# Four experts, four orders: how the second and first products of a mixture of experts are woven on TensorE

## The chip, the core and the metric

The kernel runs on one core of a Trainium2 chip. The metric is the device time of one execution in microseconds. Everything below the section on the profile is taken from one execution recorded by the hardware profiler.

## What is computed

Three stages follow one another: a gated linear attention, a bilinear layer, and a mixture of four experts. Cut to what matters:

```python
def reference(q, k, v, alpha, w1, w2, w3, w_out, domain_probs, e_w1, e_w2):
    for t in range(768):                       # batch 4, heads 8, head_dim 48
        state = alpha_t * state + outer(k_t, v_t)
        y_t = q_t @ state
    x = y as (3072 tokens, 384)
    x = ((x @ w1) * (x @ w2)) @ w3 @ w_out     # inner width 1024
    p = domain_probs / (domain_probs.sum(-1) + 1e-9)
    out = 0
    for e in range(4):                         # the part that the change touches
        h = maximum(x @ e_w1[e], 0)            # 384 -> 1024
        out += p[:, e] * (h @ e_w2[e])         # 1024 -> 384
```

## The kernel before, in words

**Stages.** The attention and the bilinear layer take the first 414 us. The rest, some 800 us, are the experts, and only they are changed.

**Tiling of the experts.** The 3072 tokens are six tiles of 512. For each expert (a Python loop over 4) the tiles are taken two at a time in three rounds; the first two rounds are the body of a loop on the engine (`pe.Fori`), the third is written out. A round has 16 steps: two tiles, and for each the eight blocks of 128 of the inner width. All values are fp32, and each product is made of three: every operand is split into a high and a low part, and high x high, one low x high and the other high x low are added up in the same bank of PSUM.

**The first product (line 1175, `up2_product`), "U" below.** For one tile and one block of 128 inner columns: 3 blocks of the model width by 3 terms, 9 matmuls of 512 columns. They gather in bank 0 or 1 by the step's parity. The ninth releases ScalarE, which writes `h_hi` as the relu (line 601), and that releases VectorE, which writes `h_lo`, the rest (line 821).

**The second product (line 1294, `down2_product`), "D" below.** For the same tile and block: four groups of 128 tokens by 3 terms, 12 matmuls of 384 columns. Group `sub` gathers in bank 5, 2, 3 or 4 (`SUM_BANKS`; bank 5 is one of `score_banks` in the profile's names) over the eight steps of a tile. After the last, VectorE multiplies by the gate and adds to `total` (line 1000), and counts up `added`; the first D of the next tile in that bank waits for it (line 1291).

**The order (line 1299, `step2`).** Step s makes the D of block s and, in between, the U of step s + 2, so that ScalarE and VectorE have a whole step for h. TensorE waits at the head of a step for `h_lo` of the step, and at a tile's first block for the loaded activations (`up2_waits`). Within the step the Python loop writes D number i and, where i % 4 is 1, 2 or 3, a U behind it. As there are 12 D and 9 U, the step is three times the same seven: D D U D U D U. Read as a ring (the seventh is followed by the first), such a pattern of four D and three U can take five different forms. The last two steps of all have no U.

**Other engines.** ScalarE and POOL also split the weights of the next expert in pieces; the queue on SP loads activations and weights, each load behind a count of finished U or D, and stores `total` during the last expert. Their code is not changed.

Of the kernel before, what the change touches and what calls it, by code (L numbers as in the profile page):

```python
# [31 lines left out]
BATCH, HEADS, SEQ, D = 4, 8, 768, 48  # L32
# [11 lines left out]
KT, FT = DM // P, FF // P  # L44
# [11 lines left out]
SUBS = TILE2 // P  # L56
# [9 lines left out]
FOLD_BANKS = [0, 1, 2, 3, 4, 0, 1, 2]  # L66
SUM_BANKS = [5, 2, 3, 4]
TERMS = 3
assert KT * TERMS == SUBS * TERMS - TERMS
WARM = 6  # L70
CONSTANTS = 7
FLAG_STEP = STEPS1 - 4
# [16 lines left out]
def gated_attention_experts(nc, akq, v, akq_long, v_columns, w3T, w_out, wsets, probs, out):  # L89
# [4 lines left out]
    with ExitStack() as ctx:  # L94
# [924 lines left out]
        def _(pe):  # L1019
# [143 lines left out]
            def up2_waits(e, m, s):  # L1163
                u, f = divmod(s, FT)
                if f == 0:
                    pe.wait_ge(x1_loaded[u], 32 * (e * ROUNDS + m + 1))
                    if u == 0 and isinstance(m, int) and m == 0:
                        pe.wait_ge(piece_lo, PIECES * (e + 2))

            def up2_product(e, s, i):  # L1170

                u, f = divmod(s, FT)
                k, term = divmod(i, TERMS)
                cols = slice(k * FF + f * P, k * FF + (f + 1) * P)
                mm = pe.matmul(bank[s % 2][:, :], (we_hi if term < 2 else we_lo)[e % 2][:, cols], (x1_lo if term == 1 else x1_hi)[u][:, k, :],  # L1175
                               start=(i == 0), stop=(i == KT * TERMS - 1))
                if i == KT * TERMS - 1:
                    mm.then_inc(up_done, 1)
# [36 lines left out]
            for k in range(FT):  # L1215
# [5 lines left out]
                for f in range(FOLD_FIRST):  # L1221
# [5 lines left out]
                    else:  # L1227
                        i = k - SPLIT_FROM
# [55 lines left out]
            def down2_product(e, m, s, i):  # L1284

                u, f = divmod(s, FT)
                sub, term = divmod(i, TERMS)
                if term == 0 and e == 0 and s == 0 and sub >= 1:
                    pe.wait_ge(x1_lo_ready, X1_LOW_AHEAD + KT * (TILES1 * BATCH - 1) + sub)
                if term == 0 and f == 0:  # L1290
                    pe.wait_ge(added, SUBS * (e * TILES2 + 2 * m + u) + sub + 1)
                rows = slice(sub * P, (sub + 1) * P)
                cols = slice(KT * FF + f * DM, KT * FF + (f + 1) * DM)
                mm = pe.matmul(bank[SUM_BANKS[sub]][:, 0:DM], (h_hi if term < 2 else h_lo)[:, s % 2, rows], (we_lo if term == 1 else we_hi)[e % 2][:, cols],  # L1294
                               start=(f == 0 and term == 0), stop=(f == FT - 1 and term == TERMS - 1))
                if f == FT - 1 and term == TERMS - 1:
                    mm.then_inc(down_done, 1)

            def step2(e, m, s, ahead):

                pe.wait_ge(h_lo_ready, STEPS2 * (e * ROUNDS + m) + s + 1)
                if ahead:
                    up2_waits(*ahead)
                ups = 0
                for i in range(SUBS * TERMS):
                    down2_product(e, m, s, i)
                    if ahead and i % SUBS >= 1:
                        up2_product(ahead[0], ahead[2], ups)
                        ups += 1

            def round2(e, m, following):

                for s in range(STEPS2):
                    if s + 2 < STEPS2:
                        step2(e, m, s, (e, m, s + 2))
                    else:
                        step2(e, m, s, following and (*following, s + 2 - STEPS2))
# [64 lines left out]
```

## Time and profile before

| | |
|---|---|
| Median of 3 runs | 1219.2 us (1218.31 to 1219.39) |
| Span of the profiled execution | 1217.6 us, 18865 instructions |
| TensorE matmuls (PE) busy | 1212.3 us, 100%, 7740 matmuls |
| TensorE weight loads (PEld) busy | 1118.6 us, 92% |
| VectorE (DVE) busy | 461.4 us, 38% |
| ScalarE (ACT) busy | 281.7 us, 23% |
| GpSimd (POOL) busy | 168.8 us, 14% |

How to read it: the span is the time from the first to the last instruction on the core; each engine's busy time is a share of it, and engines work side by side. PE is the matmul, PEld the load of its stationary operand, which runs beside the matmul before. The chain of waits starts at the last instruction and goes back to what released each one. The records of consecutive matmuls overlap each other, so TensorE's busy time can't be divided by the number of matmuls.

### The profile page before, as it was taken

How to read it: one execution, taken by the hardware profiler on the slowest of the kernel's cores; microseconds unless marked ns; L12 is line 12 of the kernel's file. 1: busy time of each engine (PE TensorE's matmuls, PEld its weight loads, DVE VectorE, ACT ScalarE, POOL GpSimd, SP SyncE). 2: the span in 40 equal slices, each digit the busy share in tenths (PEclk: the TensorE clock that was granted, in tenths of full speed). 3: DMA queues.
4: the chain of work that ended last, by engine and by line, in shares of the span. 5: the costliest groups of instructions: out<-in, count | busy, mean ns of one | idle time of the engine just before them, and what ended most of it. 6: DMA issues, size and time to landing. Idle time of an engine off the chain costs nothing.

```text
span 1217.6 us, 18865 instructions
## 1 busy us (share of the span) xinstructions
PE 1212.3 (100%) x7740; PEld 1118.6 (92%) x7740; DVE 461.4 (38%) x886; ACT 281.7 (23%) x526; POOL 168.8 (14%) x148
## 2 busy tenths in 40 slices
PE   9999999999999999999999999999999999999998
PEld 8799999999999999999999999999999999999998
DVE  6997586586651122122222222222122222222222
ACT  3443333333333311111111111111111111111111
POOL 1132222222223520000000000000000000000000
PEclk9999999999999999999999999999999999999999
DMA  9644444544415331100141111123101111222201
GB/s 286 207 121 122 126 132 106 137 128 105 126 47 195 106 145 52 51 17 36 53 156 52 52 52 52 52 73 135 42 15 46 52 52 53 78 78 78 78 9 44
DMA packets 87543, 108.03 MB, mean 89 GB/s; under 512 B 38576, under 2 KB 57904, under 8 KB 86960
## 3 DMA queue, kind: packets, MB, share of 16 engines
q1 hardware_dynamic: 87184, 106.63, 28.0%
q8 instruction: 52, 0.85, 0.3%
q10 hardware_dynamic: 288, 0.39, 0.1%
q14 instruction: 19, 0.16, 0.0%
HBM read 86.29 MB, written 18.35 MB: 86 GB/s over the span
## 4 chain that ended last, share of the span: by engine, by line
PE 99%; DVE 0%; issue 0%; DVEq 0%; ACT 0%
PE bank L1175 33%; PE bank L1294 25%; PE bank L1022 9%; PE bank L1024 9%; PE bank L1023 9%; PE score_banks L1294 8%; PE bank L1063 2%; PE bank L1244 1%; PE score_banks L1084 1%; PE bank L1073 1%; PE score_banks L1047 1%; PE bank L1226 1%; PE bank L1214 0%; DVE total L1000 0%; PE bank L1031 0%
## 5 line engine op out<-in xcount | busy, mean ns | idle before, releaser
L821 DVE SCALAR_TENSOR_TENSOR h_lo<-bank,h_hi 128x512 fp32r<-128x512 f32 x192 | 132.8, 691 | 584.9 <-ACT h_hi L601 584.0
L601 ACT ACTIVATE h_hi<-bank 128x512 fp32r<-128x512 f32 x192 | 114.7, 597 | 661.7 <-PE bank L1175 661.7
L1175 PE MATMUL bank<-x_hi,we_lo 128*128 128x512 f32 x576 | 228.7, 397 | 0.0
L1175 PE MATMUL bank<-x_hi,we_hi 128*128 128x512 f32 x576 | 224.1, 389 | 0.0
L1175 PE MATMUL bank<-x_lo,we_hi 128*128 128x512 f32 x576 | 223.5, 388 | 0.0
L1294 PE MATMUL bank<-we_hi,h_hi 128*128 128x384 f32 x576 | 194.6, 338 | 0.0
L1294 PE MATMUL bank<-we_lo,h_hi 128*128 128x384 f32 x576 | 194.5, 338 | 0.0
L1294 PE MATMUL bank<-we_hi,h_lo 128*128 128x384 f32 x576 | 193.8, 336 | 0.0
L499 POOL TENSOR_TENSOR we_lo<-we_raw,we_hi (+1 forms) x48 | 60.9, 1289 | 527.8 <-ACT we_hi L562 527.8
L1175 PEld LDWEIGHTS bank<-x_hi,we_lo 128*128 128x128 f32 x576 | 108.3, 188 | 22.4
L1175 PEld LDWEIGHTS bank<-x_lo,we_hi 128*128 128x128 f32 x576 | 108.0, 188 | 22.7
L1022 PE MATMUL bank<-x,wb_hi 128*128 128x384 f32 x384 | 128.6, 335 | 0.0
L1024 PE MATMUL bank<-x,wb_lo 128*128 128x384 f32 x384 | 128.3, 334 | 0.0
L1023 PE MATMUL bank<-x,wb_hi 128*128 128x384 f32 x384 | 128.3, 334 | 0.0
L1294 PEld LDWEIGHTS bank<-we_hi,h_hi 128*128 128x128 f32 x576 | 108.3, 188 | 8.5
L1294 PEld LDWEIGHTS bank<-we_hi,h_lo 128*128 128x128 f32 x576 | 108.3, 188 | 8.4
L1175 PEld LDWEIGHTS bank<-x_hi,we_hi 128*128 128x128 f32 x576 | 108.3, 188 | 0.2
L1294 PEld LDWEIGHTS bank<-we_lo,h_hi 128*128 128x128 f32 x576 | 108.1, 188 | 0.0
L510 POOL TENSOR_TENSOR g_lo<-g_sb,g_hi 128x384 fp32r<-128x384 f32 x64 | 66.3, 1036 | 221.3 <-ACT g_hi L591 221.3
L811 DVE TENSOR_TENSOR g_sb<-a_sb,bank 128x384 f32<-128x384 f32 x64 | 35.3, 552 | 110.8 <-PE bank L1024 110.8
L1022 PEld LDWEIGHTS bank<-x,wb_hi 128*128 128x128 f32 x384 | 72.1, 188 | 0.2 <-issue 0.2
L1023 PEld LDWEIGHTS bank<-x,wb_hi 128*128 128x128 f32 x384 | 72.1, 188 | 0.1
(99 smaller groups left out, 1473.3 us busy)
## 6 DMA issues: line engine op xcount, KB each, us to landing
x_hi<-x_hi_spill SPq DMA_DIRECT2D x24, 768.0 KB, 4.8
x_lo<-x_lo_spill SPq DMA_DIRECT2D x24, 768.0 KB, 6.3
we_raw<-wset SPq DMA_DIRECT2D x4, 3072.0 KB, 10.0
inputs<-akq SPq DMA_DIRECT2D x24, 448.0 KB, 5.2
values<-v_rows SPq DMA_DIRECT2D x24, 256.0 KB, 3.7
inputs<-akq SPq DMA_DIRECT2D x24, 224.0 KB, 3.3
x_hi_spill<-x_hi_out SPq DMA_DIRECT2D x8, 576.0 KB, 4.3
x_lo_spill<-x_lo_out SPq DMA_DIRECT2D x8, 576.0 KB, 5.2
```

Of the source, the lines that this page charges most:

```text
L499: pool.tensor_tensor(set_lo(n)[:, at], set_raw(n)[:, at], set_hi(n)[:, at], ALU.subtract).then_inc(piece_lo, 1)
L510: pool.tensor_tensor(g_lo[:, s % 2, :], g_sb[:, s % 2, :], g_hi[:, s % 2, :], ALU.subtract).then_inc(g_lo_ready, 1)
L601: act.activation(h_hi[:, s % 2, :], bank[s % 2][:, :], ACT.Relu).then_inc(h_hi_ready, 1)
L811: dve.tensor_tensor(g_sb[:, s % 2, :], a_sb[:, s % 2, :], bank[1][:, 0:TILE1], ALU.mult).then_inc(g_ready, 1)
L821: dve.scalar_tensor_tensor(out=h_lo[:, s % 2, :], in0=bank[s % 2][:, :], scalar=0.0, in1=h_hi[:, s % 2, :], op0=ALU.max, op1=ALU.subtract) ...
L1022: pe.matmul(dst, left[0], right[0], start=first, stop=False)
L1023: pe.matmul(dst, left[0], right[1], start=False, stop=False)
L1024: return pe.matmul(dst, left[1], right[0], start=False, stop=last)
L1047: mm = pe.matmul(bank[5 + half][rows, STATE_AT + i * D:STATE_AT + (i + 1) * D], keys_t[:, pair, rows], values[:, c % SLOTS, at], start=(i ...
L1063: mm = pe.matmul(bank[7][q * ODD:(q + 1) * ODD, (2 * row + g) * CHUNK:(2 * row + g + 1) * CHUNK], values[:, c % SLOTS, at], scores[:, row, ...
L1175: mm = pe.matmul(bank[s % 2][:, :], (we_hi if term < 2 else we_lo)[e % 2][:, cols], (x1_lo if term == 1 else x1_hi)[u][:, k, :], start=(i ...
L1294: mm = pe.matmul(bank[SUM_BANKS[sub]][:, 0:DM], (h_hi if term < 2 else h_lo)[:, s % 2, rows], (we_lo if term == 1 else we_hi)[e % 2][:, cols],
```

## The change

The order of D and U within a ring becomes a string of seven letters for each expert, repeated three times for a step. Each expert gets another one of the four forms of a ring that the old order is not. The matmuls, their operands, their count, the order of the D among themselves and of the U among themselves, and the waits at the head of the step stay the same. In a step without U the letters U are passed over.

```diff
@@ -66,7 +66,8 @@
 TERMS = 3
-assert KT * TERMS == SUBS * TERMS - TERMS
+ORDERS = [weave * TERMS for weave in ("DDDDUUU", "DUDDDUU", "DUUDDDU", "DDUDDUU")]
+assert all((weave.count("D"), weave.count("U")) == (SUBS * TERMS, KT * TERMS) for weave in ORDERS)
@@ -1301,10 +1302,12 @@
                 pe.wait_ge(h_lo_ready, STEPS2 * (e * ROUNDS + m) + s + 1)
                 if ahead:
                     up2_waits(*ahead)
-                ups = 0
-                for i in range(SUBS * TERMS):
-                    down2_product(e, m, s, i)
-                    if ahead and i % SUBS >= 1:
+                ups = downs = 0
+                for product in ORDERS[e]:
+                    if product == "D":
+                        down2_product(e, m, s, downs)
+                        downs += 1
+                    elif ahead:
                         up2_product(ahead[0], ahead[2], ups)
                         ups += 1
```

Counted over a ring, with the seventh product followed by the first:

| order | experts | D then D | U then U | D then U |
|---|---|---|---|---|
| DDUDUDU | all, before | 1 | 0 | 3 |
| DDDDUUU | 0 | 3 | 2 | 1 |
| DUDDDUU | 1 | 2 | 1 | 2 |
| DUUDDDU | 2 | 2 | 1 | 2 |
| DDUDDUU | 3 | 2 | 1 | 2 |

## Rows read from the trace of the kernel before

**Rows 1.** The page: busy time and share by engine, and shares of the chain.
```profile
PE 1212.3 (100%) x7740; PEld 1118.6 (92%) x7740; DVE 461.4 (38%) x886; ACT 281.7 (23%) x526; POOL 168.8 (14%) x148
...
PE 99%; DVE 0%; issue 0%; DVEq 0%; ACT 0%
```

**Rows 2.** Chain (start, length, what); between them busy time by engine, clock 1.00.
```profile
421.28 0.35 PE bank L1294 x2
...
1208.91 0.35 PE bank L1294 x2
...
421.28:1208.91 787.63, 787.63 (x3978) 717.87 (x3977) 185.32 (x281) 131.60 (x225) 53.47 (x37) 1.00 0.18 63
```

**Rows 3.** Timeline of matmuls (start us, us, engine, line): one ring.
```profile
800.03 0.39 PE L1175 MATMUL bank<-x_hi,we_hi 128*128 128x512 f32 x1
800.25 0.34 PE L1294 MATMUL bank<-we_hi,h_hi 128*128 128x384 f32 x1
800.43 0.39 PE L1175 MATMUL bank<-x_lo,we_hi 128*128 128x512 f32 x1
800.66 0.34 PE L1294 MATMUL bank<-we_lo,h_hi 128*128 128x384 f32 x1
800.83 0.40 PE L1175 MATMUL bank<-x_hi,we_lo 128*128 128x512 f32 x1
801.07 0.34 PE L1294 MATMUL bank<-we_hi,h_lo 128*128 128x384 f32 x1
...
801.41 0.39 PE L1175 MATMUL bank<-x_hi,we_hi 128*128 128x512 f32 x1
```

**Rows 4.** Same view: nine U before the stage, and what follows.
```profile
413.76 0.39 PE L1175 MATMUL bank<-x_hi,we_hi 128*128 128x512 f32 x1
...
414.21 0.40 PE L1175 MATMUL bank<-x_hi,we_lo 128*128 128x512 f32 x1
414.45 0.40 PE L1175 MATMUL bank<-x_hi,we_hi 128*128 128x512 f32 x1
...
415.85 0.34 PE L1022 MATMUL bank<-g_hi,wp_hi 128*128 128x384 f32 x1
...
416.54 0.33 PE L1023 MATMUL bank<-g_lo,wp_hi 128*128 128x384 f32 x1
```

**Rows 5.** Same view: D of the last two steps, without U.
```profile
1210.48 0.34 PE L1294 MATMUL score_banks<-we_hi,h_lo 128*128 128x384 f32 x1
...
1211.20 0.33 PE L1294 MATMUL bank<-we_hi,h_hi 128*128 128x384 f32 x1
...
1212.93 0.33 PE L1294 MATMUL bank<-we_lo,h_hi 128*128 128x384 f32 x1
```

**Rows 6.** The same view: first ring of the stage.
```profile
419.91 0.34 PE L1294 MATMUL score_banks<-we_lo,h_hi 128*128 128x384 f32 x1
...
420.31 0.34 PE L1294 MATMUL score_banks<-we_hi,h_lo 128*128 128x384 f32 x1
420.48 0.40 PE L1175 MATMUL bank<-x_lo,we_hi 128*128 128x512 f32 x1
...
421.29 0.34 PE L1294 MATMUL bank<-we_hi,h_lo 128*128 128x384 f32 x1
```

**Rows 7.** Timeline: a step's first D, VectorE's h_lo, the next step's first D.
```profile
802.45 0.34 PE L1294 MATMUL score_banks<-we_hi,h_hi 128*128 128x384 f32 x1
...
803.28 0.69 DVE L821 SCALAR_TENSOR_TENSOR h_lo<-bank,h_hi 128x512 fp32r<-128x512 f32 x1 [3.47 <-ACT h_hi L601]
...
806.61 0.34 PE L1294 MATMUL score_banks<-we_hi,h_hi 128*128 128x384 f32 x1
```

**Rows 8.** Timeline at a tile's end: VectorE's last addition, and the tile's last D.
```profile
453.13 0.62 DVE L1000 SCALAR_TENSOR_TENSOR total<-bank,gate,total 128x384 f32 x1 [0.36 <-PE bank L1294]
...
452.61 0.34 PE L1294 MATMUL bank<-we_hi,h_lo 128*128 128x384 f32 x1
```

**Rows 9.** Timeline of VectorE: last activations of the bilinear stage.
```profile
418.19 1.49 DVE L816 TENSOR_TENSOR x_lo_out<-bank,x_hi_out 128x384 fp32r<-128x384 f32 x3 [0.82 <-ACT x_hi_out L597]
```

## The prediction

> **What bounds the kernel now.** I read the page's busy times first, then the chain of waits, then the experts' stage product by product. TensorE is busy over the whole span, and of the chain that ended last 99% are its own instructions [rows 1]; in the experts' stage the granted clock is 1.00, the level of 2.4 GHz [rows 2]. The changed code is the experts' stage: "D" is one second product (line 1294, 384 columns, 128x384) and "U" one first product (line 1175, 512 columns, 128x512). A step has 12 D and 9 U, woven as three rings of seven, now D D U D U D U. There are 4 experts x 3 loop rounds x 16 steps = 192 steps, of which the last two have no U, so 190 x 3 = 570 rings. The chain shows the same piece, the two neighbouring D that open a ring, at 421.28 and at 1208.91 us; between them lie 3978 matmul records, 568 rings of seven but for the edges [rows 2]. So a ring takes 787.63 / 568 = 1.3867 us, and nowhere in the stage is there idle time to win: 570 rings are 790.4 us, 65% of the span. The change can act only through this number, or by opening a wait that isn't there now. The execution profiled has a span of 1217.6 us; the median of the runs is 1219.2, so 1.6 us lie around the span, and I add to the median what I work out.
>
> **Starts, not durations.** Records of consecutive matmuls overlap: a D is written with 0.34 us and a U with 0.39 or 0.40, yet the next one starts after 0.17 to 0.24 [rows 3]. What a product costs is the distance from its start to the next start. (The Trainium skill, Perfetto Trace Analysis, on the TensorE instruction: the end that the profiler gives is computed from the size of the instruction. The trace agrees, since the recorded durations of a ring add up to 2.5 us against 1.39.)
>
> **What a ring is made of.** In one ring in the middle of the stage the starts are 800.03 (U), 800.25 (D), 800.43 (U), 800.66 (D), 800.83 (U), 801.07 (D), another D, and again U at 801.41 [rows 3]. The distances, rounded to 10 ns, are 0.22, 0.18, 0.23, 0.17, 0.24, and 0.34 for the two D together: D takes 0.17 to 0.18 and U 0.22 to 0.24. Two pure sequences stand beside it.
> - Pure U: nine in a row at 413.76 to 415.85, 2.09 us [rows 4], 232 ns each. They aren't even: the first two take 0.45 (225 to 230 ns each), the first three 0.69, and the last six 1.40, 233 ns each. The 384-column products that follow (line 1022 to 1024) run at once at 0.17: four of them take 0.69.
> - Pure D: of the last 24, the ten from 1211.20 to 1212.93 take 1.73, 173 ns each [rows 5]; but the third to sixth after the last ring take 1211.20 - 1210.48 = 0.72, 180 each.
>
> **The change part by part.** It removes and adds no instruction. Number and size of the products are the same, so are the sums that each bank gathers, and the waits at the head of a step stay there. What moves is how often like follows like. A ring (cyclic) has now one D-D, no U-U, and three changes each way. Expert 0 (DDDDUUU) gets three D-D, two U-U, one change each way; experts 1 to 3 get two D-D, one U-U, two changes each way, with D in runs of 1 and 3 or of 2 and 2, and U in runs of 1 and 2.
>
> Pure rates first: 4 D at 173 and 3 U at 233 are 1392 ns, 5 above the ring of now. With the U at the 225 to 230 of the first two of a run it would be 1367 to 1382. The mixed ring lies between, so part of the U's excess is not paid when D's lie among them. Whether it matters where they lie is what the trace has to say.
>
> Expert 0, from the nearest rows: three U that begin a run after 384-column products took 0.69, and four 384-column products after a run of U took 0.69 [rows 4], together 1.38 us within rounding, the ring of now. (The run before them was long, the ring's D run has four; with a run of U at its settled pace the ring is 3 x 233 + 4 x 173.5 = 1393.) Price: between -7 (rounding) and +7 ns by 144 rings, -1.0 to +1.0 us; I take +0.2.
>
> Experts 1 to 3, 426 rings: no U-U pair between D's exists in the trace, so bounds. Low: the pair at 0.455, the single U at 0.226, D at 0.174: 1377, -10 ns. High: pair at 0.467, single U at the settled pace of the run too, 0.233, which is about what the dearest one in the ring shows, D at 0.174: 1396, +9 ns. This is -4.1 to +4.0 us. I take the middle, near 0, by one more set of rows. The first ring of the stage, counted from its second product because the first one waits, runs from 419.91 to 421.29, 1.38 us, and in it the D between the first and the second U takes 0.17, from 420.31 to 420.48 [rows 6]. In the settled ring the D in that place takes 0.18, from 800.25 to 800.43 [rows 3]. The starts fall otherwise by some ns (near what the rounding of 10 ns lets one see) and the total stays. That looks like a pace that holds over a ring, within which starts shift by some ns, and not like a fixed price for each neighbour. Sum: +0.2 + 0.1 = +0.3 us.
>
> **Waits of the step's head, cost nothing.** A step's D need the h of their step. VectorE's h_lo, which follows ScalarE's h_hi, begins at 803.28, when the step before has been running since 802.45, and takes 0.69, so it is ready at 803.97. The step that reads it starts at 806.61: 2.6 us early [rows 7]. The last product of a step is a U in the old and all the new orders, so what releases ScalarE doesn't move against the step. Cover gone, a step would wait; but 2.6 us is longer than any reordering within a ring of 1.39.
>
> **Banks of the sums.** On each tile's last step VectorE adds each bank to `total`, the last starting at 453.13 after the D at 452.61, 0.62 long, done at 453.75 [rows 8]. Bank 3 of the sums is written again by the tenth D of the next step. From the last D to the end of its step are a D and a U, 0.40, so that step starts at 453.01; the earliest that any new order brings the tenth D is the first place of its third ring, 2 x 1.387 later, 455.8: 2.0 us to spare. The fourth D (second bank) comes forward from the sixth place to the fourth in expert 0, 0.4 us, but that bank's last D and its addition come two groups, over half a step of 4.16 us, before the last bank's. VectorE's adds end before the h_lo that queues behind them on its engine. In the very first step the fourth D also waits for the halves of the last activations: VectorE's three subtractions run from 418.19 for 1.49, until 419.68 [rows 9], and the second D of that step starts at 419.91 [rows 6], so the fourth can't come before it. No wait. The DMA queue on SP waits for counts of finished first or second products of a whole tile, which shift by less than a ring.
>
> **A rule that would not see the order.** The ring shows a gap of 0.22 to 0.24 for 512 columns and 0.17 to 0.18 for 384 [rows 3]. The Trainium skill (TensorE: Matmul & The Clock Gate, Back-to-back issue gap) gives columns / 2.4 + 2.5 ns, for any order. An estimate by that page: 4 x 162.5 + 3 x 215.8 = 1297 ns for a ring, old or new, so a change of 0; the trace shows 1387, so there is a part of 13 ns per product that this rule lacks and that could depend on neighbours.
>
> **The rivals.**
> - Each neighbour has its price, on the dear side (slower). Where U meet they run at the settled 233, and in a run of D the third and fourth take the 180 of rows 5 in place of 174. Expert 0: 2 D more at +6 and U at 233, +7 from the pure rates, so +19 x 144 = +2.7 us. The others: +6 for the third D (two orders of three) and +3 for the pair: about +7 x 426 = +3.0. Together +5.7, 1224.9; with the U-U alone about +2.5, 1221.7. For it: rows 4 and 5 show both paces. Against: after the nine U the D show no slow third and fourth. It is above the bound of 0.2% (2.4 us) from about 4.3 ns per ring on.
> - The isolated U is the dear one (faster). In the ring of now a U costs up to 0.24 although it has D on both sides, and at the head of a run only 0.225 to 0.23. If fewer changes mean fewer late starts, experts 1 to 3 get 1377: -4.1 us, expert 0 -1.0: 1214.1. Against: the settled run of U is no cheaper than the dear single one.
> - A wait opens (slower): one of the covers above would have to be wrong by 2 us. If it were one per tile with 0.5 us, 24 tiles cost 12 us, 1231. Nothing in the rows speaks for it.
> - The order isn't kept in the program, or TensorE evens it out: same, 1219.2. TensorE's queue has no other order in the records than the code's, so this falls together with the forecast.
>
> **How the numbers follow.** Forecast, ring conserved: 54%, 1219.5, its own range 1217.5 to 1221.5. Neighbours' price: 27%, 1221.7 to 1224.9, of which a little (3%) stays within the bound. Isolated U dear: 17%, 1214 to 1217, with 1% in the bound. A wait: 2%. A measurement of this kernel tells 0.2% (2.4 us) from no change. Faster 0.16, same 0.58, slower 0.26. The range reaches into both rivals, 1214.8 to 1225.0.
>
> **What would show it.** The ring in each of the four experts, from the chain or the starts: 1387 +-3 ns if right; in expert 0 near 1406 and in the others near 1394 if neighbours have their price; 1377 in experts 1 to 3 if the isolated U was dear. The three U of expert 0 should start 0.69 us before the next D, the four D take 0.69 to 0.70. VectorE's idle before h_lo (3.47 us a step, [rows 7]) and no wait of TensorE in the stage should stay. A different ring in each of experts 1 to 3, though they have the same counts of neighbours, would show that the place and not the count matters, and make the working wrong.

## The result

| | before | changed |
|---|---|---|
| median of the runs of the two kernels on one chip (11 each) | 1218.71 us | 1221.87 us |
| lowest to highest | 1218.27 to 1219.67 | 1220.60 to 1223.18 |
| span of the profiled execution | 1217.6 us | 1220.2 us |

The ratio is 1.0023, with a 95% interval of 1.0015 to 1.0032: slower. The medians differ by 3.2 us (0.26%), a little over the 0.2% that a measurement of this kernel can tell from no change.

The page of the changed kernel (line numbers are one higher than before: first products L1176, second products L1295) shows the engines as they were. The lines answer to [rows 1]:

```profile
PE 1214.9 (100%) x7740; PEld 1117.4 (92%) x7740; DVE 461.1 (38%) x886; ACT 282.0 (23%) x526; POOL 169.0 (14%) x148
...
PE 99%; DVE 0%; issue 0%; DVEq 0%; ACT 0%
```

TensorE is busy 2.6 us longer with the same 7740 matmuls, and the span is 2.6 us longer. The waits in the experts' stage (who waited <- for whom: us in total, times, longest) have no wait of TensorE in them but the 0.4 us of the stage's very first product, which the kernel before has too:

```profile
ACT h_hi L602 <- PE bank L1176: 661.4, 191, 3.8
DVE h_lo L822 <- ACT h_hi L602: 588.4, 185, 3.7
...
PEld score_banks L1295 <- DVEq L1011: 0.4, 1, 0.4
```

So the time went into the distances between matmuls that wait for nothing. An easy instrument for that is a stretch of fixed length inside each expert and the count of matmul records in it. Four stretches of 180 us, one per expert, first of before, then of the changed kernel (stretch, its length, TensorE's busy time and records, granted clock, DMA share, GB/s):

```profile
430.00:610.00 180.00, 180.00 (x910) 1.00 0.15 53
630.00:810.00 180.00, 180.00 (x911) 1.00 0.13 44
830.00:1010.00 180.00, 180.00 (x910) 1.00 0.13 44
1025.00:1205.00 180.00, 180.00 (x911) 1.00 0.16 57
```
```profile
430.00:610.00 180.00, 180.00 (x902) 1.00 0.15 53
630.00:810.00 180.00, 180.00 (x910) 1.00 0.13 44
830.00:1010.00 180.00, 180.00 (x909) 1.00 0.13 44
1025.00:1205.00 180.00, 180.00 (x911) 1.00 0.16 57
```

Records that only reach into a stretch are counted too, about two each time, so 902 stands for 900 products, 7 x 180 / 900 = 1.400 us a ring. Expert 0 is the slow one, expert 2 is one or two products short, experts 1 and 3 are as before. From the start of each expert's first D to the next expert's, the trace gives it to the nanosecond ("ring" is the mean over all its rings but the first of the stage, which holds the wait):

| expert | order now | before, us | now, us | difference | ring now, ns |
|---|---|---|---|---|---|
| 0 | DDDDUUU | 199.791 | 201.711 | +1.920 | 1400.1 |
| 1 | DUDDDUU | 199.680 | 199.671 | -0.009 | 1386.6 |
| 2 | DUUDDDU | 199.679 | 200.162 | +0.483 | 1390.0 |
| 3 (46 steps with U) | DDUDDUU | 191.360 | 191.364 | +0.004 | 1386.7 |

Together +2.40 us of the span's +2.56. The rest, 0.17 us, is that this execution reached the first D that much later (419.79 against 419.62 us). The medians differ by 3.16 us, and the interval of the ratio is 1.8 to 3.9 us, in which 2.4 lies. Most of the other 0.8 is the choice of executions: the profiled one of the kernel before took 1219.39 us, 0.7 over its median, and that of the changed kernel 1221.87, its median.

**Expert 0 from close by.** Its rings take 1387 and 1413 ns by turns. The timeline shows two of them, one from 421.29 to 422.70 (1.41) and one from there to 424.09 (1.39):

```profile
421.29 0.34 PE L1295 MATMUL bank<-we_lo,h_hi 128*128 128x384 f32 x1
421.46 0.34 PE L1295 MATMUL bank<-we_hi,h_lo 128*128 128x384 f32 x1
421.64 0.34 PE L1295 MATMUL bank<-we_hi,h_hi 128*128 128x384 f32 x1
421.81 0.35 PE L1295 MATMUL bank<-we_lo,h_hi 128*128 128x384 f32 x1
422.00 0.40 PE L1176 MATMUL bank<-x_hi,we_hi 128*128 128x512 f32 x1
...
422.70 0.34 PE L1295 MATMUL bank<-we_hi,h_lo 128*128 128x384 f32 x1
...
423.40 0.39 PE L1176 MATMUL bank<-x_hi,we_hi 128*128 128x512 f32 x1
423.62 0.39 PE L1176 MATMUL bank<-x_lo,we_hi 128*128 128x512 f32 x1
423.85 0.40 PE L1176 MATMUL bank<-x_hi,we_lo 128*128 128x512 f32 x1
424.09 0.34 PE L1295 MATMUL score_banks<-we_hi,h_hi 128*128 128x384 f32 x1
```

In the dear ring the four D take 0.71 (the last 0.19) and the three U 0.70, in the cheap one 0.70 and 0.69. The unrounded distances, in ns, in a pair of rings later in the expert: 175 175 177 185 234 232 235, then 174 174 175 174 226 229 235. The cheap ring is the one that the prediction put together from [rows 4]. The dear one has in its third and fourth D the slow products of [rows 5], and all its U at the settled pace of a long run.

### The profile page after: what moved, and what is told of

Read it like the earlier page. It is cut to its first block, busy times and chain, and to the rows that moved or that the text cites. A ratio compares the mean times of both kernels' runs of the same rounds, so it can differ in the third digit from the quotient of the medians.

```text
span 1220.2 us, 18865 instructions
## 1 busy us (share of the span) xinstructions
PE 1214.9 (100%) x7740; PEld 1117.4 (92%) x7740; DVE 461.1 (38%) x886; ACT 282.0 (23%) x526; POOL 169.0 (14%) x148
## 4 chain that ended last, share of the span: by engine, by line
PE 99%; DVE 0%; issue 0%; DVEq 0%; ACT 0%
PE bank L1176 33%; PE bank L1295 25%; PE bank L1023 9%; PE bank L1025 9%; PE bank L1024 9%; PE score_banks L1295 8%; PE bank L1064 2%; PE bank L1245 1%; PE score_banks L1085 1%; PE bank L1074 1%; PE score_banks L1048 1%; PE bank L1227 1%; PE bank L1215 0%; DVE total L1001 0%; PE bank L1032 0%
## 5 line engine op out<-in xcount | busy, mean ns | idle before, releaser
L1176 PE MATMUL bank<-x_hi,we_lo 128*128 128x512 f32 x576 | 226.9, 394 | 0.0
L1176 PE MATMUL bank<-x_hi,we_hi 128*128 128x512 f32 x576 | 226.3, 393 | 0.0
L1176 PE MATMUL bank<-x_lo,we_hi 128*128 128x512 f32 x576 | 225.7, 392 | 0.0
L1295 PE MATMUL bank<-we_hi,h_lo 128*128 128x384 f32 x576 | 193.9, 337 | 0.0
L1295 PE MATMUL bank<-we_hi,h_hi 128*128 128x384 f32 x576 | 193.9, 337 | 0.0
L1295 PE MATMUL bank<-we_lo,h_hi 128*128 128x384 f32 x576 | 193.6, 336 | 0.0
L1295 PEld LDWEIGHTS bank<-we_hi,h_lo 128*128 128x128 f32 x576 | 108.1, 188 | 14.4
L1295 PEld LDWEIGHTS bank<-we_hi,h_hi 128*128 128x128 f32 x576 | 108.3, 188 | 12.6
L1176 PEld LDWEIGHTS bank<-x_hi,we_hi 128*128 128x128 f32 x576 | 108.1, 188 | 12.2
L1295 PEld LDWEIGHTS bank<-we_lo,h_hi 128*128 128x128 f32 x576 | 108.2, 188 | 11.9
L1176 PEld LDWEIGHTS bank<-x_hi,we_lo 128*128 128x128 f32 x576 | 108.1, 188 | 6.4
L1176 PEld LDWEIGHTS bank<-x_lo,we_hi 128*128 128x128 f32 x576 | 108.0, 188 | 0.2
```

## The experiments

Three theories were formed after the result. **A:** the order alone sets the length of the ring. **B:** the place does, that is which expert it is, with what runs beside it and comes before it. **C:** each neighbour has its price, so orders with equal counts of neighbours are equal. Later theories are named where they come up. All ring lengths are worked out from starts, as in the table above.

### One order in all experts: DDDDUUU

```diff
-ORDERS = [weave * TERMS for weave in ("DDDDUUU", "DUDDDUU", "DUUDDDU", "DDUDDUU")]
+ORDERS = [weave * TERMS for weave in ("DDDDUUU",) * EXPERTS]
```

> All four experts get DDDDUUU, the order that only expert 0 has in the changed kernel. There its ring takes 1401 ns in the mean against 1387 before. If the order alone sets the ring (theory A): all four experts show about 1400, 570 rings x 13.3 ns = +7.6 us, about 1226.3 against 1218.7. If it is the place, that is what runs beside expert 0 or the transition from the stage before (theory B): 1400 in expert 0 only and 1387 in the others, about 1220.7. If the price is per neighbour (theory C): as theory A, since all rings have the same neighbours.

Measured: 1227.39 us, ratio 1.0066 (1.0049 to 1.0083) to the kernel before, measured beside it at 1219.46: +7.9 us. Its four stretches:

```profile
430.00:610.00 180.00, 180.00 (x901) 1.00 0.15 53
630.00:810.00 180.00, 180.00 (x902) 1.00 0.13 44
830.00:1010.00 180.00, 180.00 (x902) 1.00 0.14 47
1025.00:1205.00 180.00, 180.00 (x901) 1.00 0.16 57
```

All four experts are now as slow as expert 0 was; the rings are 1400.0 to 1400.1, by turns about 1387 and 1413, in each. B is out: the expert, and what runs beside it, has no part in it. From the rings 13.3 x 570 = 7.6 us are expected; from the first D to the last matmul the trace has 802.10 us against 794.53 before, 7.57 more.

### One order in all experts: DUDDDUU

The same line with "DUDDDUU".

> All four experts get DUDDDUU, the order of expert 1 alone in the changed kernel, whose ring there takes 1386.6 ns. Theory A (the order alone): 1386.7 in all four and the time of the kernel before, 1218.7 to 1219.0. Theory B (the place): expert 0 near 1400 and expert 2 near 1390 whatever their order, about 1221. Theory C (each neighbour has its price, two D-D and one U-U): all three orders with these counts give one and the same ring.

Measured: 1219.25 us, ratio 1.0001 (0.9992 to 1.0011). The ring is 1386.7 in all four experts. Two of its stretches:

```profile
430.00:610.00 180.00, 180.00 (x910) 1.00 0.15 51
630.00:810.00 180.00, 180.00 (x911) 1.00 0.13 44
```

### One order in all experts: DUUDDDU

The same line with "DUUDDDU".

> All four experts get DUUDDDU, the order of expert 2 alone in the changed kernel, whose ring there takes 1390.0 ns, by turns 1382 and 1398. Theory A: 1390 in all four, 570 x 3.3 = +1.9 us, 1220.6. Theory B: 1400 in expert 0, 1390 in expert 2, 1387 in 1 and 3, about 1221.2. Theory C: the same ring as DUDDDUU and DDUDDUU in the same call, which have the same counts of neighbours; a difference between them of over 1 ns per ring ends it.

Measured: 1220.88 us, ratio 1.0009 (1.0000 to 1.0019), +1.4 us where 1.9 was expected; in the trace, from the first D to the last matmul, 796.40 us against 794.53 before, +1.87. The ring is 1390.0 in all four experts, by turns 1382 and 1398. Its stretches hold one to three records less than the 910 and 911 of DUDDDUU:

```profile
430.00:610.00 180.00, 180.00 (x909) 1.00 0.15 53
630.00:810.00 180.00, 180.00 (x908) 1.00 0.13 44
```

The two orders have the same counts: two D-D, one U-U, two changes each way. C is out, and with it the prediction's rival of that form. The two rings are mirror images of each other, so the direction matters.

### One order in all experts: DDUDDUU

The same line with "DDUDDUU".

> All four experts get DDUDDUU, the order of expert 3 alone in the changed kernel, whose ring there takes 1386.7 ns. Theory A: 1386.7 in all four, 1218.7 to 1219.0. Theory B: 1400 in expert 0 and 1390 in expert 2, about 1221. Theory C: the same ring as the two other orders with two D-D and one U-U.

Measured: 1218.66 us, ratio 0.9994 (0.9984 to 1.0004); the ring is 1386.7 in all four. Three of the five possible orders have exactly the same ring, though their products start at quite different distances: 174 175 227 180 226 172 233 in the old order, 174 176 234 173 168 227 235 in this one. In these three orders a D followed by a U takes 168 to 180, depending on where it stands.

### First products of 384 columns, in the old order and in DDDDUUU

```diff
-                mm = pe.matmul(bank[s % 2][:, :], ..., (x1_lo if term == 1 else x1_hi)[u][:, k, :],
+                mm = pe.matmul(bank[s % 2][:, 0:wide], ..., (x1_lo if term == 1 else x1_hi)[u][:, k, 0:wide],
```

with `wide` 384 for the woven products and 512 for the two sets ahead of the stage.

> The kernel before with the order DDUDUDU, but every woven first product computes only 384 of its 512 columns (the last 128 tokens of each tile are left out). All products then have the width at which pure runs take 173.3 ns. If the excess over columns / 2.4 + 13.3 ns comes from products of two widths next to each other, or from 512 columns: the ring is 7 x 173.3 = 1213 ns and every distance 173 to 174, whatever the order; time about 1218.7 - 570 x 0.1733 = 1120. If it comes from changing between the two kinds of product (their banks, their operands), a ring takes more than 1217.

> The kernel with DDDDUUU in all four experts, with the woven first products cut to 384 of 512 columns as in the run before it. If the loss of 13.3 ns per ring hangs on the 512 columns: ring 1213 ns as in the old order at 384 columns, no difference of the two, about 1120. If it hangs on long runs of the same kind (the same bank time after time, or the same operands' memory): the ring stays about 13 ns over that of the old order at this width, near 1227.

Measured: 1124.47 and 1124.44 us, one execution each, spans of 1122.7 us for both, the ring 1220.0 in every expert of both. The chain of DDDDUUU (start, length, what) shows D and U now alike:

```profile
501.25 0.52 PE bank L1176 x3
501.77 0.70 PE bank L1295 x4
502.47 0.52 PE bank L1176 x3
502.99 0.70 PE bank L1295 x4
```

At equal widths of 384 these two orders cost the same. That isn't shown for the others: at 448 columns (below) the same two are equal again, and two other orders differ from them. The ring isn't the 1213 of seven products at the pure pace of D either; 6.7 ns stay. In both kernels the D behind the last U of a ring takes 180, in the old order it alone of the three D that stand behind a U. That the mixing of the two kinds makes these 6.7 ns is not shown, as no pure run of U at 384 columns is on record.

### The middle term into another bank

```diff
-mm = pe.matmul(bank[s % 2][:, :], ..., start=(i == 0), stop=(i == KT * TERMS - 1))
+mm = pe.matmul(bank[s % 2 if term != 1 else 6 + s % 2][:, :], ..., start=(i <= 1), stop=(i >= KT * TERMS - 2))
```

> DDDDUUU in all experts at full width, but the middle term of the first products gathers in another bank (6 or 7) and is left out of the result, so that no two first products in a row write the same bank. If the loss of DDDDUUU comes from first products following each other in one bank: the ring falls from 1400 to 1387. If it has nothing to do with the bank: 1400 stays, by turns 1387 and 1413.

Measured: 1226.63 us in one execution, span 1224.9, as DDDDUUU in all experts; the ring 1400, by turns 1387 and 1413. One stretch:

```profile
630.00:810.00 180.00, 180.00 (x901) 1.00 0.13 44
```

That first products follow each other in one bank of PSUM is not the cause. The second products, which gather by threes in one bank, were left as they were.

### Twelve second products, then nine first ones

```diff
+ORDERS = ["D" * SUBS * TERMS + "U" * KT * TERMS for _ in range(EXPERTS)]
```

> Each step makes its twelve second products and then its nine first products, a ring of 21 in place of three of seven. If the loss comes once per long run (runs of D pay what a run of U left behind, as the D at the end of the kernel before did with 28 ns over six products): about 12 x 173.3 + 9 x 232 + up to 28 = 4168 to 4200 ns a step against 3 x 1386.7 = 4160 before and 3 x 1400 = 4200 for DDDDUUU, so 1220 to 1226. If the loss grows with each first product that follows another: 12 x 173.3 + 9 x 233.3 and the excess of the ring of DDDDUUU, over 4200, above 1226.

Measured: 1222.98 us in one execution (1218.46 for the kernel before beside it), span 1221.2; a step takes 4173.3 ns, 1391 for a third of it. The stretches show 908 records each:

```profile
630.00:810.00 180.00, 180.00 (x908) 1.00 0.13 44
```

The longest runs that a step allows cost 13.3 ns a step over the old order, a third of the 40 that runs of four and three cost. The distances are 174 174 175 and then 173 for D, and 226 229 235 232 235 232 235 ... for U, step after step; the slow third and fourth D are not there. So neither the length of a run nor the number of U-U pairs is what is paid. Of the two forms expected the first has the right number, at its low end, but not for its reason: it had the D pay for the run of U, and here the D are at 174 and the nine U at 232 each.

### Rings of several orders in a step

```diff
+ORDERS = [
+    "DDDDUUU" + "DDUDUDU" * 2,
+    "DDDDDDDDUUUUUU" + "DDDDUUU",
+    "DUUDDDU" + "DUDDDUU" + "DDUDUDU",
+    "DDDDUUU" * 2 + "DDUDUDU",
+]
```

> Steps of 21 products with different rings in them, by expert: (0) DDDDUUU DDUDUDU DDUDUDU, (1) DDDDDDDDUUUUUU DDDDUUU, (2) DUUDDDU DUDDDUU DDUDUDU, (3) DDDDUUU DDDDUUU DDUDUDU. A step of the old order takes 4160.0 ns, of DDDDUUU 4200.0, of twelve D and nine U 4173.3. If each DDDDUUU costs its mean of 13.3 ns wherever it stands (theory P): (0) 4173, (3) 4187. If the loss is a slip of 26.7 ns that needs two such rings in a row, as they cost 0 and 26.7 by turns (theory Q): (0) 4160, (3) 4187. (1): two runs of each kind, 4187 if the loss is once per pair of runs, as twelve and nine cost 13.3 in one. (2): DUUDDDU is 1382 and 1398 by turns; if its good turn could be had alone, 4155, under the old order; if the excess is a pace over more than a ring, 4160 to 4163.

Measured, a step by expert: 4180.0, 4193.3, 4160.0, 4186.6 ns, where the old order has 4160.0. The one execution took 1222.24 us and the one of the kernel before beside it 1222.02, which is too close to read; in the trace the stretch from the first D to the last matmul is 798.31 us against the 794.53 of the kernel before. The stretches:

```profile
430.00:610.00 180.00, 180.00 (x906) 1.00 0.15 51
630.00:810.00 180.00, 180.00 (x903) 1.00 0.13 44
830.00:1010.00 180.00, 180.00 (x911) 1.00 0.13 44
1025.00:1205.00 180.00, 180.00 (x904) 1.00 0.16 57
```

A ring DDDDUUU costs 20 ns where rings of the old order come before and after it (expert 0), and a second one behind it 6.7 more (expert 3). Neither P (13.3 each) nor Q (nothing for one alone) holds for one alone; for two in a row Q and P both gave 4187. Expert 1, with two runs of each kind, is at 33.3 over the old order where 27 were expected. What a run of four D costs depends on what stood before it: behind a ring of the old order its D take 174 176 177 185 and its U 234 232 235, behind another dear one 173 174 175 174 and 225 230 235. Expert 2 shows that the cheap turn of DUUDDDU (1382) can't be had alone: its ring takes 1398 there, the two good orders behind it 1379 and 1384, and the step 4160.0 again, the same as three rings of any good order.

### First products of 448 columns

The edit of the 384-column kernels with 448, and four orders, one per expert.

> The woven first products compute 448 of 512 columns (the last 64 tokens of each tile are left out). Orders by expert: DDDDUUU, DDUDUDU, DUUDDDU, DUDDDUU. A floor of columns / 2.4 + 13.3 is 4 x 173.3 + 3 x 200 = 1293.3 ns per ring. At 512 the three best orders stand 13.3 over that floor and DDDDUUU 26.7; at 384 both orders tried stand 6.7 over it. If the excess grows with the difference of the widths: the best orders at about 1303, DDDDUUU at about 1310. If 512 columns (a full bank) are what is dear: all four at 1300, as at 384.

Measured: 1175.48 us in one execution; by expert 1313.4 ns (DDDDUUU), 1313.3 (DDUDUDU), 1306.7 (DUUDDDU), 1306.7 (DUDDDUU), from steps of 3940 and 3920. Stretches of 170 us:

```profile
430.00:600.00 170.00, 170.00 (x908) 1.00 0.16 56
620.00:790.00 170.00, 170.00 (x908) 1.00 0.14 47
810.00:980.00 170.00, 170.00 (x912) 1.00 0.14 47
990.00:1160.00 170.00, 170.00 (x913) 1.00 0.17 61
```

Neither of the two expectations holds. The old order, one of the best at 512 columns, is as slow as DDDDUUU here, and 20 ns over the floor (the expectation's 1293.3) where it was 13.3 over it at 512; DUUDDDU, second to last there, is among the best.

### Second products of 512 columns

```diff
+                at = KT * FF + f * DM
+                cols = slice(at, at + (TILE2 if f < FT - 1 else DM))
```

> Second products of seven of the eight blocks of a tile compute 512 columns in place of 384 (the last 128 are not used; the result is the same). All products of those steps then have one width. Orders by expert: DDDDUUU, DDUDUDU, DUUDDDU, DUDDDUU. If the loss of DDDDUUU needs two widths in a ring (theory W1): all four experts show one ring in these steps, near 7 x 233 = 1633 ns, the pace of the pure run of 512. If it hangs on 512 columns following each other (theory W2): a ring is then all such products, equally 1633 in all four, but above seven times 227 = 1587 by the full excess. If it hangs on the kind of product (banks, operands) and not on width: DDDDUUU stays 13 ns above the others.

Measured: 1337.98 us in one execution; a ring in the steps with 512 columns: 1613.3 (DDDDUUU), 1626.7 (DDUDUDU), 1623.3 (DUUDDDU, in the mean), 1630.0 (DUDDDUU, in the mean). Stretches of 210 us, in which one step of eight has the narrow D:

```profile
430.00:640.00 210.00, 210.00 (x926) 1.00 0.13 44
660.00:870.00 210.00, 210.00 (x920) 1.00 0.11 38
890.00:1100.00 210.00, 210.00 (x923) 1.00 0.12 38
1110.00:1320.00 210.00, 210.00 (x919) 1.00 0.14 49
```

All three forms expected fall. The orders differ with all widths equal (against W1 and W2), and the kind of product doesn't make DDDDUUU slow either: it is now the fastest of the four, 13 ns below the old order. The kind isn't without effect, though: in that ring the second to fourth D take 226 to 227 and the U 231 to 235, at one width. Each order ran in one expert only here and at 448 columns; that the place has no part was shown at the kernel's own widths.

### The two orders undone

```diff
+ORDERS = [weave * TERMS for weave in ("DDUDUDU", "DUDDDUU", "DDUDUDU", "DDUDDUU")]
```

> The changed kernel with the order of experts 0 and 2 put back to DDUDUDU; experts 1 and 3 keep DUDDDUU and DDUDDUU. Theory A (the order alone sets the ring, 1400 for DDDDUUU, 1390 for DUUDDDU, 1386.7 for the other three): all four experts at 1386.7 ns a ring, a time equal to before, 1218.7 to 1219.4, ratio 1.000 within 0.1%. If experts 1 or 3 cost anything outside their rings (a later start of the stage, a longer end), it stays above before by part of the 3.2 us of the changed kernel.

Measured: 1218.66 us, ratio 0.9999 (0.9990 to 1.0008), the kernel before beside it 1218.94. The span is 1217.6 us, the ring 1386.7 in all four experts, and the stretches are those of before but for one record:

```profile
430.00:610.00 180.00, 180.00 (x910) 1.00 0.15 53
630.00:810.00 180.00, 180.00 (x910) 1.00 0.13 44
830.00:1010.00 180.00, 180.00 (x910) 1.00 0.13 44
1025.00:1205.00 180.00, 180.00 (x911) 1.00 0.16 57
```

The whole loss of the changed kernel hangs on the orders of experts 0 and 2. No kernel with the same products is faster than the one before by more than the measurement can tell.

## Why the prediction was right or wrong

**The time.** The forecast was 1219.5 us, no change; it became 1221.87, slower by 0.23%. It lies within the range given, but outside the forecast's own range of 1217.5 to 1221.5, and on the side of the rival, with its chance of 26%.

**The term that was mis-sized: expert 0.** It was priced at -1.0 to +1.0 us, with +0.2 taken, and is +1.92. The step that failed is the joining of rows of [rows 4]: three U at the head of a run (0.69) and four narrow products behind a run of U (0.69), both from long pure runs, taken as if one ring could have both every time. It has both every second time. In between comes a ring with 26.7 ns more. The upper end failed too. It was made of pure rates, 1393, and the mean is 1400: the slow third and fourth D of [rows 5] had been read, but were put into a rival and left out of the bound. Unrounded, those two D take 178 and 185. With them (+4 and +11 ns) and the U at 233 a ring comes to about 1409, near the dear one's 1413.

**Experts 1 to 3.** Taken near 0, between -4.1 and +4.0 us; measured +0.48. The middle and the reason for it held for three of the orders: one total (1386.7), with starts distributed otherwise. For DUUDDDU, and more so for DDDDUUU, the total isn't kept. "A pace that holds over a ring" was thus half of it; its one support, [rows 6], was a ring of the old order behind a wait, not another order. The runs with other widths show that the total isn't a property of the products alone.

**The rival with a price per neighbour** named the right side and the right rows, and gave 1406 and 1394 for the rings. Measured were 1400 and 1387 to 1390; the mechanism is wrong, since DUUDDDU and DUDDDUU have equal neighbours and differ by 3.3 ns, and twelve and nine in a row cost less than four and three. Its full sum, 2.7 us for expert 0 and 3.0 for the others, is too high in both parts (1.92 and 0.48). That the measured time lies just inside 1221.7 to 1224.9 is luck: the low end, by the U-U price alone, has expert 0 too low and the others too high.

**The rival with a dear isolated U** didn't happen: no order at the kernel's widths has a ring under 1386.7 in the mean.

**The waits.** As written: no wait of TensorE in the stage, and undoing two orders gives back the whole time. In the changed kernel's trace h_lo is at least 2.6 us early at every step but the last, where it is 0.6, as before. The banks of the sums are free at least 1.7 us before they are written again, a little less than the 2.0 of the prediction. (That 2.0 has a slip on the safe side: the product at the first place of a step's third ring is the ninth D, not the tenth.)

**The last sentence of the prediction** said that different rings in experts 1 to 3, which have the same counts, would show that the place and not the count matters. They differ (1386.6, 1390.0, 1386.7), so this sign of being wrong came, by 3.3 ns in one order. The place that matters is that of a product in the sequence; the expert has no part.

## What to carry to other kernels

Where TensorE is never idle, the order of its products can still have a price, here 0 to 13 ns in the mean on a ring of 1.39 us, and it couldn't be added up from prices of pairs taken from pure runs; the distances of starts have to be measured over two periods of the pattern at least, since rings can alternate. Counting the matmul records in stretches of equal length is enough to see 0.2%. And a best order holds for the widths at which it was found: with all products at 512 columns the slowest order became the fastest of the four that ran.

## What the runs showed of the hardware

Take as a floor columns / 2.4 plus 13.3 ns a product, from the 173.3 ns of pure runs of 384 columns (and it fits the cheapest U of the old ring, 226 to 227). The excess over it, for a ring of four D and three U, in ns:

| columns of U, D | floor | DDDDUUU | DDUDUDU | DUUDDDU | DUDDDUU | DDUDDUU |
|---|---|---|---|---|---|---|
| 384, 384 | 1213.3 | 6.7 | 6.7 | not run | not run | not run |
| 448, 384 | 1293.3 | 20.0 | 20.0 | 13.3 | 13.3 | not run |
| 512, 384 | 1373.3 | 26.7 | 13.3 | 16.7 | 13.3 | 13.3 |
| 512, 512 | 1586.7 | 26.7 | 40.0 | 36.7 | 43.3 | not run |

Most are multiples of 6.7 ns; the three that aren't (16.7, 36.7, 43.3) are means over rings or steps of two lengths by turns. The floor isn't the pace of every pure run: the last six of nine U of 512 columns take 233.3 each [rows 4], 6.7 over it. The granted clock was 1.00 in all of the stretches. The Trainium skill (TensorE: Matmul & The Clock Gate, Back-to-back issue gap) has columns / 2.4 + 2.5 ns for a product by itself, without a term for what stands beside it. In these runs it is 13.3 in place of 2.5 in a pure run of 384 columns, and a mixed ring has 1 to 6 ns more a product, in part by the order.

**What stays open** is what makes the excess. It is not that first products follow each other in one bank of PSUM, not a wait, not the length of runs alone, not a difference of widths alone, not what other engines do in an expert. That one ring changes what the next one costs (1387 and 1413 by turns; four D behind an old ring 177 and 185, behind a dear one not) shows that something carries over from product to product. The records of the weight loads don't show what: in the experts' stage each begins 2 to 4 ns after the start of the product before it, in the kernel before and in the changed one alike. Whether it is how far TensorE is ahead in reading operands is a guess that no run here tests. Which operands the two kinds read, and at which addresses, was never varied.
